# Two held-back product blocks in groups 1 and 2, 256 columns in groups 4 and 5, products of the identity in three norms

## What is computed

```python
for t in range(S):
    cur = einsum('bhd,bhe->bhde', u * k_t, v_t)
    y[t] = einsum('bhd,bhde->bhe', r_t, state + cur)
    state = w_t[..., None] * state + einsum('bhd,bhe->bhde', k_t, v_t)
x = y as [B, S, 384]
h = relu(x @ w_in)                       # 384 -> 1024
conv_out[t] = sum over 3 taps of conv_w[k] * h[t + k - 1]
x = (h * sigmoid(conv_out)) @ w_out      # 1024 -> 384
xn = (x - mean) / sqrt(var + 1e-6) * g_ln
out = x + relu(xn @ w_ch1) @ w_ch2       # 384 -> 1536 -> 384
```

## Time and profile before

| | us |
|---|---|
| median of 3 runs | 356.25 |
| the three runs | 355.31, 356.25, 358.69 |
| profiled execution, its time | 356.21 |
| profiled execution, its span | 354.5 |
| TensorE busy | 333.5 (94%) |
| VectorE busy | 247.6 (70%) |
| ScalarE busy | 145.1 (41%) |
| GpSimd busy | 74.1 (21%) |
| mean granted TensorE clock | 0.995 |

### The profile page before, as it was taken

The page is one execution under the profiler, slowest core; times in us unless marked ns, Lnnn a source line. Parts: engine busy times, 40 slices in busy tenths (PEclk is TensorE's granted clock), DMA queues, the critical chain, the costliest instruction groups (busy, mean ns, idle before and its releaser), DMA issues.

```text
span 354.5 us, 8508 instructions
## 1 busy us (share of the span) xinstructions
PE 333.5 (94%) x3193; PEld 313.1 (88%) x3193; DVE 247.6 (70%) x523; ACT 145.1 (41%) x351; POOL 74.1 (21%) x138
## 2 busy tenths in 40 slices
PE   6877988999999799999899999899999999998996
PEld 6766867999999699999699999699999999997996
DVE  4997997977878767669779479767786612685212
ACT  2215984544266311266412157421265421663220
POOL 5633001144330222130205130204200030000300
PEclk9999998999999999999999999999999999999999
DMA  9998362822243610245305523501000010000101
GB/s 153 203 247 227 125 186 70 156 69 44 31 85 47 113 24 2 31 50 104 64 3 91 70 44 62 96 3 24 2 1 3 2 44 2 0 3 0 47 0 44
DMA packets 89251, 22.79 MB, mean 64 GB/s; under 512 B 83423, under 2 KB 87674, under 8 KB 89210
## 3 DMA queue, kind: packets, MB, share of 16 engines
q1 hardware_dynamic: 87984, 21.84, 30.6%
q10 hardware_dynamic: 1226, 0.41, 0.6%
HBM read 19.87 MB, written 2.36 MB: 63 GB/s over the span
## 4 chain that ended last, share of the span: by engine, by line
PE 80%; DVE 8%; issue 3%; SPq 3%; DMA 2%; POOL 2%; ACT 1%; DVEq 0%; POOLq 0%; ACTq 0%
PE hid L582 12%; PE hid L586 11%; PE hid L583 11%; PE acc L594 10%; PE acc L595 9%; PE acc L602 4%; PE acc L601 4%; PE pair_a L1320 2%; PE y_ps L1357 2%; DVE cg L1039 2%; SPq L695 2%; DVE stats L1219 2%; DVE cg L1223 1%; PE y_ps L1363 1%; PE y_ps L1369 1%
## 5 line engine op out<-in xcount | busy, mean ns | idle before, releaser
L1018 ACT ACTIVATE g_hi<-hid 128x256 fp32r<-128x256 f32 x64 | 24.6, 384 | 106.2 <-PE acc L602 94.1
L1250 DVE SCALAR_TENSOR_TENSOR g_lo<-hid,g_hi 128x256 fp32r<-128x256 f32 x64 | 26.8, 419 | 51.7 <-ACT g_hi L1018 51.5
L582 PE MATMUL hid<-xc_hi,w_hi 128*128 128x256 f32 x216 | 55.4, 288 | 2.5 <-ACT xc_hi L998 2.3
L583 PE MATMUL hid<-xc_hi,w_lo 128*128 128x256 f32 x216 | 53.0, 277 | 0.0
L1039 DVE SCALAR_TENSOR_TENSOR cg<-h_all,cols,cg 128x256 f32<-128x256 f32 x96 | 47.0, 490 | 6.2 <-ACT cg L967 5.5
L582 PEld LDWEIGHTS hid<-xc_hi,w_hi 128*128 128x128 f32 x216 | 40.6, 188 | 5.5 <-ACT xc_hi L998 3.7
L594 PE MATMUL acc<-w_hi,g_hi 128*128 128x384 f32 x128 | 43.9, 343 | 0.0
L595 PE MATMUL acc<-w_lo,g_hi 128*128 128x384 f32 x128 | 43.1, 337 | 0.0
L583 PEld LDWEIGHTS hid<-xc_hi,w_lo 128*128 128x128 f32 x216 | 40.6, 188 | 0.0
L582 PE MATMUL hid<-x_hi,win_hi 128*128 128x258 f32 x144 | 37.6, 289 | 1.0 <-ACT x_hi L928 1.0
L583 PE MATMUL hid<-x_hi,win_lo 128*128 128x258 f32 x144 | 36.8, 283 | 0.0
(11 more groups left out here) (188 smaller groups left out, 765.5 us busy)
## 6 DMA issues: line engine op xcount, KB each, us to landing
v_in<-in_v SPq DMA_DIRECT2D x12, 192.0 KB, 4.0
lent<-in_moe_w_ch SPq DMA_DIRECT2D x6, 384.0 KB, 3.2
out<-x SPq DMA_DIRECT2D x10, 192.0 KB, 1.9
lent<-in_moe_w_in SPq DMA_DIRECT2D x6, 256.0 KB, 4.5
lent<-in_moe_w_out SPq DMA_DIRECT2D x4, 384.0 KB, 5.8
w_two<-in_w SPq DMA_DIRECT2D x6, 192.0 KB, 4.9
k_two<-in_k SPq DMA_DIRECT2D x6, 192.0 KB, 5.1
ruk<-in_r SPq DMA_DIRECT2D x6, 192.0 KB, 2.9
```

The costliest lines, as they stand in the source:

```text
L582: pe.matmul(out_ps, wh, xh, start=i == 0, stop=False)
L583: pe.matmul(out_ps, wl, xh, start=False, stop=False)
L1018: act.activation(relu_parts(n, j)[0], hid[j % 2][:, 0:GP], ACT.Relu)\
L1250: dve.scalar_tensor_tensor(out=low, in0=hid[j % 2][:, 0:GP], scalar=0.0, in1=high.bitcast(F32), op0=ALU.max, op1=ALU.subtract).then_inc(s_ ...
```

## The change

- Group 1 and group 2 hold back two blocks each (`LATE_OF`), with new tiles `mid_hi`, `mid_lo`; groups 3 and 4 still hold back four. `HELD_FROM` is 2, so groups 2 to 5 sum their first half in `pair_a`, `pair_b`. Scores of tiles 8 to 11 and these sums alternate in the banks: `sc` waits until ScalarE has copied the sums (`summed`), `project` until the scores are masked (`masked`). There is one score buffer from tile 6 on, so `mask` n waits for `y` n - 1. The second output buffer is a weight stage that is free by then.
- Hidden blocks of groups 4 and 5 compute 256 columns. GpSimd keeps the last two columns of each hidden block of groups 3 and 4 (`h_kept`) and puts them in front of the same block of the next group; ScalarE's middle tap waits for that (`s_back`).
- VectorE makes the output in one instruction a tile for groups 1 to 5; `project2` 0 of the next group and the 1 / std of the next group wait for it (`s_out`).
- TensorE runs 34 transposes of the identity into unused columns of `y_ps`, ahead of waits in the norms of groups 0, 1 and 5 (`FILL`).
- `FIRST` and `AFTER` are written anew.

```diff
-        LATE = 4
-        HELD_FROM = GROUPS - 2
+        LATE_OF = {1: 2, 2: 2, 3: 4, 4: 4}
+        HELD_FROM = 2
...
+        mid_hi = [sb(f"mid_hi{i}", [P, GP], F32R) for i in range(2)]
+        mid_lo = [sb(f"mid_lo{i}", [P, GP], F32R) for i in range(2)]
...
         def held(g, j):
-            return HELD_FROM - 1 <= g < GROUPS - 1 and j >= J2 - LATE
+            return j >= J2 - LATE_OF.get(g, 0)
...
+        def masked(g):
+            return 2 * sum(p[0] == "sc" for p in ORDER[:ORDER.index(("project", g, 0))])
+
+        def summed(item):
+            sums = [p[1] for p in ORDER[:ORDER.index(item)] if p[0] == "project" and p[1] >= HELD_FROM]
+            if not sums:
+                return 0
+            assert ("norm", sums[-1]) in ORDER[:ORDER.index(item)]
+            return G * (sums[-1] + 1)
...
         AFTER = {
...
-            ("conv", 0, 7): [("weights", 12), ("weights", 13)],
-            ("gate", 0, 7): [("w", 3)],
+            ("conv", 0, 7): [("weights", 12), ("k", 3)],
+            ("project", 0, 5): [("weights", 13), ("w", 3)],
+            ("project", 0, 6): [("r", 3)],
             ("norm", 0): [("ke", 2)],
-            ("turn", 0): [("r", 3), ("load_w", 5), ("scan1", 3)],
+            ("turn", 0): [("scan1", 3)],
...
-            ("project", 2, 7): [("x", 7)],
-            ("norm", 2): [("row_r", 8), ("row_r", 9), ("kv", 7)],
+            ("project", 2, 5): [("x", 7)],
+            ("project", 2, 7): [("late", 1, 10), ("late", 1, 11)],
+            ("turn", 2): [("kv", 7), ("k", 8)],
...
+            ("hidden", 3, 1): [("kv", 8), ("state", 8)],
...
+            ("norm", 3): [("late", 2, 10), ("load_v", 10), ("x", 9), ("ru", 10), ("late", 2, 11)],
+            ("turn", 3): [("kv", 9), ("ruk", 10)],
...
+        def begins(g):
+            return g < 4 or g * G % SEQ == 0
+
+        def ends(g):
+            return g < 3 or (g + 1) * G % SEQ == 0
...
+                elif kind == "hidden":
+                    if not begins(n):
+                        pool.wait_ge(s_g, q - HBUFS + 1)
+                        pool.wait_ge(s_kept, kept(n - 1, j))
+                        pool.tensor_copy(h[:, 0:2], h_kept[:, j, :]).then_inc(s_back, 1)
+                    if not ends(n):
+                        pool.wait_ge(s_h, q + 1)
+                        if not begins(n):
+                            pool.wait_ge(s_back, returned(n, j))
+                        pool.tensor_copy(h_kept[:, j, :], h[:, GP:WIN]).then_inc(s_kept, 1)
...
+                        act.activation(h_sb[q % HBUFS][:, 2:WIN], hid[j % 2][:, 0:GP], ACT.Relu).then_inc(s_h, 1)
...
+                    if not begins(n):
+                        act.wait_ge(s_back, returned(n, j))
...
-                elif kind == "result" and n == GROUPS - 1:
+                elif kind == "result" and n > 0:
...
+            FILL = {("turn", 0, 0): 6, ("turn", 0, 1): 4, ("hidden2", 0, 0): 3,
+                    ("turn", 1, 0): 7, ("turn", 1, 1): 4, ("hidden2", 1, 0): 3,
+                    ("turn", 5, 1): 4, ("hidden2", 5, 0): 3}
+
+            def fill(item):
+                for _ in range(FILL.get(item, 0)):
+                    pe.matmul(y_ps[:, HD:HD + P], ident[:, :], ident[:, :], start=False, stop=False,
+                              is_transpose=True, skip_group_check=True)
...
+                    new = slice(0 if begins(n) else 2, WIN)
+                    last = hidden_passes(pe, hid[j % 2][:, 0:WIN - new.start],
...
+                                           x_hi[s][:, a, new], x_lo[s][:, a, new]) for a in range(KD)],
...
                         if n >= HELD_FROM:
-                            pe.wait_ge(s_scaled, G * n)
+                            pe.wait_ge(s_out, G * n)
```

## The result

| | before | after |
|---|---|---|
| median, 16 runs each | 358.02 us | 354.71 us |
| lowest and highest | 355.31, 360.55 | 354.26, 355.88 |
| profiled execution: span | 354.5 | 352.7 |
| its mean granted clock | 0.995 | 1.000 |

The ratio is 0.992, with a 95% interval from 0.990 to 0.995: 0.8% faster, where 1.4% was forecast. By the spans, on which the sum was made, it is 1.8 us instead of 5.1. The three runs shown of before, 355.3 to 358.7, had hidden how widely that kernel spreads; the kernel after hardly spreads at all. Both facts turned out to belong to the answer.

The account below looks back on a forecast made before the run. The prediction took TensorE's stream of products as the bound, busy 333.5 of 354.5 us. Its terms, 3.8 + 1.1 + 0.6 - 0.4 = 5.1 us, took 356.2 to 351.1 us, range 349.0 to 355.5.

Parts of the forecast that it names:

- Late blocks, 3.8: Groups 1 and 2 run two held-back blocks in the next norm: 1.88 us gained a group, 3.8 for both.
- Group 0, 0.6: Ahead of group 0's statistics: weight piece 13 and three transposes moved, lowered clock perhaps avoided; 0.6 us gained, bounds 0 to 1.4.
- the split alone: Group 0: low part of weight piece 13 moved behind the last gated block on VectorE; 0.6 of 0.95 us gained.
- 256 columns, 1.1: Hidden blocks of groups 4 and 5, 258 to 256 columns: 0.07 us for each of 16 blocks, 1.1 us gained.
- Rival 1: Groups 4 and 5: the two columns count only as columns, so 1.1 becomes 0.1, 352.1 us; chance 0.14.
- Products of the identity, 0: 34 products in the norms of groups 0, 1 and 5 fit where TensorE waits; taken as 0, up to 0.7 lost.
- the 1.17 us ahead of the transposes: Stretch between last product and first transposes of an unfilled norm, taken as TensorE waiting, with room for identity products.
- Net of the new order, -0.4: Everything else reordered: 0.2 us gained from fewer attention interruptions against 0.6 for new small waits; net 0.4 lost.
- 0 within 0.7: The opening, up to the first hidden block: same end expected, within 0.7 us either way.
- Output sum on VectorE, 0: Groups 1 to 4: fused pair of 1.14 us just fits before project2; taken as 0, bad end 0.2 a group.
- rival 2: Groups 2 and 3: TensorE waits for gated operands, 3.4 of the 3.8 us return, 354.5 us; chance 0.21.
- rival 3: 16 blocks of groups 4 and 5: ScalarE's middle tap waits for GpSimd's returned columns, slower, 360.7 us; chance 0.07.

Follow-up runs that it names:

- experiment 9: Experiment 1's kernel with no blocks held back in groups 1 and 2: 359.97 us, 7.5 slower.
- experiment 8: Kernel after with 258 columns again in groups 4 and 5, nothing kept or returned on GpSimd: 354.58 us against 354.71.
- experiment 15: Experiment 13's kernel plus four warming products in the opening, and x_hi, x_lo in rows of 320 columns: 350.86 us, ratio to before 0.981.
- experiment 7: Experiment 1's kernel plus 26 sets of 16 products, both operands shifted by 0 to 192 bytes: 256 columns took 0.114 to 0.120 us a product.
- experiment 1: Kernel after with h_kept allocated behind xc_hi and xc_lo, which return to their old place: 352.44 us, ratio to before 0.982.
- experiment 2: Kernel before with an unused tensor of 64 bytes a partition ahead of xc_hi: 360.27 us against 358.57, ratio 1.006.
- experiment 10: Kernel after without the 34 products of the identity: 357.05 us, 2.3 slower.
- experiment 13: Experiment 1's kernel with the copy into v_mid of tile 3 moved on GpSimd ahead of the padding copies: median 352.51 us.
- experiment 3: Experiment 1's kernel plus 27 sets of 16 products at different operand places: 256 columns, weights unmoved, 0.113 us a product at 64 bytes, 0.117 to 0.120 elsewhere.
- experiment 6: Experiment 1's kernel plus 28 sets of 16 products, the first 17 in 64-byte steps: four places took 0.114 to 0.115 us a product, others 0.118 to 0.119.

## Why the prediction was wrong

It said 351.1 us and faster by over 1%. It was 354.7, inside the range, and 0.8% faster. Two things failed: the price of the 256 columns, and what was not asked of `h_kept`. That the time lies inside the range is in part luck. In the spans the gain is 3.3 us short of the forecast, in the medians only 1.8, because the clock gave back what nobody had counted. Step by step:

- **Late blocks, 3.8: right in kind, a little high.** 3.3 by experiment 9. The norm of group 2 grew by 0.46 more than worked out: the step had the wait for ScalarE's copies and not the one for VectorE's low part behind the scans. In addition the blocks keep the clock up in norm 2, which the step did not count.
- **Group 0, 0.6: right in the number.** Its first half went from 25.17 to 24.55 us; statistics start at 53.98 instead of 55.69, 1.1 of that by the opening. Part is the clock, which was 0.78 there and is 1.00. How much is left for the split alone, no run shows, since no profile of before has a full clock in that stretch.
- **256 columns, 1.1: the wrong step.** It read the 0.08 us between two blocks of different operands as the price of two columns. It was mostly the price of the place of `xc_hi`. At the place where `x_hi` lies, 256 columns gain nothing (experiment 8); at the fast one they gain 0.8 (experiment 15). Rival 1 had the right time for this term, 0.1, but not the right reason. At the fast place the two columns count for more than their length: 0.114 us, where 258 columns take 0.119 to 0.122 (experiment 7).
- **What was not in the sum: 2.3 us lost.** The edit brings in `h_kept`, 64 bytes of storage ahead of `xc_hi` and `xc_lo`. It had no term, and nothing asked what lies behind it (experiments 1 and 2). This is the larger part of the miss. No row of before could have priced it, but the two block times of the earlier trace rows that did not fit the column count held the sign.
- **Products of the identity, 0: wrong, in the kernel's favour.** In the median they are worth 2.3 us, by keeping the clock (experiment 10); even in the profile of one execution 1.3. The step looked at one profile, in which group 1's norm had a full clock, while the median was over executions with none to four falls. It also read the 1.17 us ahead of the transposes as waiting; the earlier trace rows have 0.50 of it idle, the rest is the state product. The fillers cost nothing even so: without them norms 0 and 1 were as long.
- **Net of the new order, -0.4: within 0.5 of it, but by parts that were not named.** The opening gained 1.1 us in the profile (0.1 to 1.3 over all profiles, since the opening of before ended anywhere from 31.1 to 32.0 and that of after at 30.7 to 31.1 where the clock held); 0 within 0.7 had been forecast. The second half of group 0 lost 0.5 without the place's share. The wait for `v_mid` accounts for all of that: without it the stage is 1.2 us shorter (experiment 13). Some 0.5 us between groups 1 and 4 remain unassigned, where attention work moved from one stage to another.
- **Output sum on VectorE, 0, and rivals 2 and 3:** the sums ran at 280.58 for 1.13 in group 4, and neither they nor GpSimd's 32 small copies, 0.18 to 0.44 us each, appear among TensorE's waits. Both rivals are out: the room of the late blocks was not given back, and ScalarE was not held up.

Added up in spans, from experiments with one profile each: late blocks -3.3, group 0 -0.6, opening -1.1, place +2.2, group 0's second half +0.5 (without the place's share), sum -2.3 against -1.8 measured.

## What to carry to other kernels

Before an edit is priced, compare where each operand of the long products lies before and after it: a tensor that no time depends on can move all behind it, and here 64 bytes took back more than half of a change's gain, 2.2 of 4.0 us in the spans. When two blocks of equal work differ, find out why before the difference is used as a price. And when a kernel's executions spread with the granted clock, price edits that fill idle time by the median and its spread, not by the one profile at hand.

## What was not expected of the hardware

- **The place of the moving operand.** fp32r products of 256 columns: 0.113 to 0.115 us apart when it starts 64 bytes off a multiple of 256 and the weights' slices 128 off, other engines idle or not, and at two more pairs of places in which it is 64 bytes behind the weights; 0.117 to 0.121 at the others, but for one set (experiments 3, 6 and 7). 384 columns showed 0.173 to 0.177 without a pattern. The trace gives no cause.
- The Trainium skill, "TensorE: Matmul & The Clock Gate", section "Back-to-back issue gap", gives N / 2.4 + 2.5 ns for one product by itself at the full clock. By that 256 columns would take 109 ns, an estimate from the page. The fast place shows 113 to 115, the others 117 to 121, so the trace agrees only roughly, and only for the fast one.
- **258 columns** took 0.119 to 0.122 at every place tried, 8 bytes off the fast one too.
- **A fall of the clock to 1.2 GHz lasted about 3.4 us and cost 1.2 to 1.4 us.** The windows of experiment 10 lack 0.29, 0.50 and 0.07 of the full clock over 2 us each, which is 3.4 us at half of it; the other falls ahead of the last product were as long. The falls came behind stretches like those shown, in which TensorE had stood for 0.5 to 0.9 of 2 us. Such a stretch alone doesn't bring it: the kernel after stands as long ahead of `v_mid` with the clock at 1.00.

```profile
78.00:80.00 2.00, 1.11 (x33) 1.00 0.00 0
```

- **Whether it comes varies between executions** of the kernel before. The kernel of experiment 13 had a mean clock of 0.994 or 0.995, so one fall, in all five executions, and its profile has it in the opening; the kernel of experiment 1, with the same opening, had none in five; experiment 7, with that opening once more, had one. What decides, no run here shows.
